# Routed experts of a fused attention, mixture and gated-product kernel: four full tiles of one expert moved ahead into the last routing, and the output weights split by GpSimd

## The reference, cut to what matters

```python
# 1. a gated linear recurrence over 768 steps, 4 batches x 8 heads, head size 48
state = f[:, :, t, :, None] * state + k[:, :, t] (x) v[:, :, t];  y[:, :, t] = q[:, :, t] @ state
# x = y as 3072 rows of 384
# 2. mixture of 8 experts, the two best of each row
noisy = x @ w_gate + log1p(exp(x @ w_noise)) * noise
top2  = two largest of noisy;  share = softmax(top2)
out[row] += share * (relu(x[row] @ w1[e]) @ w2[e])        # w1: 384x1024, w2: 1024x384
# 3. gated product
rms = sqrt(mean(x * x) + 1e-6);  xn = x / rms * rms_g
result = (silu(xn @ w_gate2) * (xn @ w_val2)) @ w_out2    # 384x1536, 1536x384
```

## Time and profile before

| what | value |
|---|---|
| median of 3 runs | 1334.63 us (1333.99 to 1335.31) |
| the profiled execution's own time | 1338.19 us |
| its span, first to last instruction | 1336.4 us |
| TensorE busy | 1239.8 us (93%) |
| VectorE, ScalarE, GpSimd busy | 880.5, 460.6, 443.0 us |
| mean granted TensorE clock | 0.978 |

### The profile page before, as it was taken

How to read it: one execution, slowest core, us unless ns; L and a number is a source line. 1 busy time by engine, 2 the same in 40 slices (tenths; PEclk the granted TensorE clock), 3 DMA queues, 4 the chain that set the end, 5 groups by cost and what they waited for, 6 DMA issues and landing times.

```text
span 1336.4 us, 26652 instructions
## 1 busy us (share of the span) xinstructions
PE 1239.8 (93%) x8897; PEld 1145.7 (86%) x8898; DVE 880.5 (66%) x1976; ACT 460.6 (34%) x975; POOL 443.0 (33%) x375
## 2 busy tenths in 40 slices
PE   4899999992999999999999999299999999999998
PEld 3787878772899999999999998299999999999997
DVE  6888888855778778778778778344444444444433
ACT  3555655642222222222222222332323323232321
POOL 8567787734614415060617600410101101010000
PEclk9999999996999999999999999699999999999999
DMA  8233433214413131313223320210101101010000
GB/s 304 67 102 125 136 119 110 69 49 153 181 69 136 47 135 41 141 54 122 94 91 109 127 109 21 80 36 19 36 21 34 54 1 54 18 35 18 0 19 18
DMA packets 36174, 105.44 MB, mean 79 GB/s; under 512 B 4992, under 2 KB 20352, under 8 KB 33664
## 3 DMA queue, kind: packets, MB, share of 16 engines
q1 hardware_dynamic: 26928, 55.62, 12.3%
q0 software_dynamic: 8592, 47.98, 10.2%
q10 hardware_dynamic: 576, 0.79, 0.2%
HBM read 77.83 MB, written 26.54 MB: 78 GB/s over the span
## 4 chain that ended last, share of the span: by engine, by line
PE 74%; DVE 8%; POOL 7%; issue 5%; ACT 4%; DMA 1%; another core or an unknown queue 0%; DVEq 0%; ACTq 0%; SPq 0%; POOLq 0%
PE pD L1529 13%; PE pD L1594 9%; PE pA L1594 9%; PE pS L1553 9%; PE pA L1553 8%; PE pA L1607 6%; PE pA L1343 5%; PE pA L1529 4%; PE pS L1607 3%; PE pA L1540 2%; PE pX L1509 1%; DVE W L974 1%; POOL fT L523 1%; POOL prods L558 1%; PE pD L1379 1%
## 5 line engine op out<-in xcount | busy, mean ns | idle before, releaser
L1204 DVE STREAM_TRANSPOSE pA<-pD 32x128 f32<-32x128 f32 x448 | 148.9, 332 | 54.1 <-PE pD L1529 47.9
L1284 DVE TENSOR_TENSOR gs<-pD,sig 128x384 f32<-128x384 f32 x96 | 53.5, 557 | 196.9 <-ACT sig L910 196.8
L1204 DVE STREAM_TRANSPOSE pA<-pA 32x128 f32<-32x128 f32 x432 | 143.6, 332 | 45.3 <-PE pA L1529 39.2
L692 POOL DMA_INDIRECT pair<-y_sorted,y_row x48 | 50.2, 1046 | 365.1 <-DVE z L1263 278.3
L858 ACT ACTIVATE hidH<-pA 128x512 fp32r<-128x512 f32 x110 | 66.0, 600 | 268.0 <-DVE pA L1204 263.2
L1343 PE MATMUL pA<-W 64*128 64x128 f32 x1920 | 141.8, 288 | 17.2 <-DVE W L974 11.5
L1529 PE MATMUL pD<-we,xsH 128*128 x498 | 155.5, 393 | 0.4 <-issue 0.4
L1343 PEld LDWEIGHTS pA<-W 64*128 64x128 f32 x1920 | 119.6, 191 | 36.5 <-DVE W L974 17.8
L1553 PE MATMUL pS<-we,hidH 128*128 x448 | 117.8, 344 | 2.4 <-DVE hidL L1211 2.0
L974 DVE TENSOR_TENSOR W<-W,prods 128x512 f32<-128x512 f32 (+1 forms) x120 | 97.8, 821 | 32.7 <-PE pA L1343 26.3
L910 ACT ACTIVATE sig<-pD 128x384 f32<-128x384 f32 x96 | 47.3, 492 | 208.4 <-PE pA L1594 208.2
(11 more groups left out here) (207 smaller groups left out, 2842.9 us busy)
## 6 DMA issues: line engine op xcount, KB each, us to landing
stage<-w POOLq DMA_DIRECT2D x14, 1536.0 KB, 8.8
qk<-qk_t SPq DMA_DIRECT2D x24, 512.0 KB, 3.7
xs<-x_sorted SPq DMA_DIRECT2D x55, 192.0 KB, 2.4
y_sorted<-yo SPq DMA_DIRECT2D x55, 192.0 KB, 1.9
fT<-f_t SPq DMA_DIRECT2D x12, 512.0 KB
vN<-v_n SPq DMA_DIRECT2D x24, 256.0 KB, 2.8
out<-fin SPq DMA_DIRECT2D x8, 576.0 KB, 2.8
stage<-w SPq DMA_DIRECT2D x2, 1536.0 KB, 13.7
```

The source lines that it names most:

```text
L692: pool.indirect_dma_start(out=pair[:, j, k], out_offset=None, in_=y_sorted[:, :], in_offset=bass.IndirectOffsetOnAxis(ap=y_row[:, t * TS + ...
L1204: ins = dve.transpose(by_32[1][32 * q:32 * (q + 1), :, i], by_32[0][32 * i:32 * (i + 1), :, q])
L1284: dve.tensor_tensor(gs[:], pD[:, f % 2 * 512:f % 2 * 512 + TT], sig[f % 2][:], ALU.mult).then_inc(s_u, 1)
```

## The change

Expert order. When eight of the twelve pairs have been routed, VectorE takes the expert with most rows so far. It becomes the first in turn, and expert 0 takes its place; all later tables go by turn. SyncE loads that expert's weights then, not at the start. Two thirds of 3072 rows with two choices are 4096 places, so that expert has at least 512 rows, four full tiles.

Early tiles. TensorE, ScalarE, VectorE and SyncE run tiles 0 to 3 (`EARLY`) between the last pair's attention and routing steps, in an order written out by hand. For these tiles TensorE transposes all of the hidden tile. The remaining 51 slots run as before. ScalarE and VectorE split the first weights in halves, two of them inside the last pair's body. GpSimd's first split waits for more steps of VectorE (`s_yrow` 10).

Output weights. GpSimd splits them in place of ScalarE and VectorE, in two column blocks (`outHa`, `outHb`, `outL`). The first block of 384 rows of the gated product is combined, squared and scaled tile by tile of 128, each on its own semaphore.

```diff
@@ SyncE @@
-            sp.dma_start(stage1[:], w1[0]).then_inc(s_stage, 16)
-            sp.dma_start(stage2[:], w2[0]).then_inc(s_stage, 16)
             pairs(body)
+            sp.wait_ge(s_most, 3)
+            e = sp.value_load(first_i[0:1, 0:1], min_val=0, max_val=E - 1)
+            sp.dma_start(stage1[:], w1[bass.ds(e, 1)]...).then_inc(s_stage, 16)
+            sp.dma_start(stage2[:], w2[bass.ds(e, 1)]...).then_inc(s_stage, 16)
+            for s in s_sc:
+                sp.wait_ge(s, 64 * 2)
+            for n in range(EARLY):
+                load_early(Tile(n), e)
+            store_rows(Tile(0))
+            sp.wait_ge(s_tab, TAB_COUNT)
+            clear_rows(sp, range(E))
+            for s in s_sc:
+                sp.wait_ge(s, 64 * (NP // 4))
+            sp.wait_ge(s_zero, 16 * E)
+            sp.wait_ge(s_tab, TAB)
+            wait_alone(sp, s_tx, 1)
+            load_rows(Tile(4))
@@ GpSimd @@
-            pool.wait_ge(s_tab, TAB)
-            for s in s_xs:
-                pool.wait_ge(s, 16)
+            pool.wait_ge(s_turn, 2)
             for e in range(1, E):
...
+                if e == 1:
+                    pool.wait_ge(s_y, NT)
+                    pool.wait_ge(s_yrow, 10)
+                    for s in s_sc:
+                        pool.wait_ge(s, 64 * (NP // 4))
...
+            pool.wait_ge(s_stage1, 16 * (E + 2))
+            for high, c in ((outHa, slice(0, OUT_A * DM)), (outHb, slice(OUT_A * DM, F2C * DM))):
+                split(high[:], outL[:, c], stage3[:, c], s_last)
@@ ScalarE: in body(NP - 1), and after it @@
+                if k == NP - 1:
+                    high_weights(0, 0)          # before soft_noise(r)
+                if k == NP - 1:
+                    high_weights(0, 1)          # before spread_state(a - 2)
+            take_rect(b, 5); take_keys(a); take_logit_parts(NP - 2); soft_noise(NP - 2); high_x(Tile(0))
+            high_weights(1, 0); take_y(a); spread_state(a); exp_gap(NP - 2); high_weights(1, 1)
+            rectify(Tile(0)); take_x(a); take_y(b); high_h(Tile(0), 0); high_h(Tile(0), 1); take_x(b)
+            take_logit_parts(NP - 1); high_x(Tile(1)); soft_noise(NP - 1); exp_gap(NP - 1); take_rows(Tile(0))
...
-            act.copy(outH[:], stage3[:]).then_inc(s_split0, 1)
@@ VectorE: in body(NP - 1), and after it @@
+                if k == NP - 1:
+                    low_weights(0, 0)           # before double_blocks(b, 3)
+                if k == NP - 1:
+                    low_weights(0, 1)           # before double_blocks(a, 5)
+            double_blocks(NT - 1, 5); take_ranks(NP - 3); low_x(Tile(0)); top2(NP - 2); new_state(NT - 2)
+            mark_chosen(NP - 2); mark_hits(NP - 2); running_counts(NP - 2); take_rows(NP - 3)
+            low_weights(1, 0); low_weights(1, 1); order_experts(); low_h(Tile(0), 0); low_h(Tile(0), 1)
+            take_ranks(NP - 2); low_x(Tile(1)); add_noise(NP - 1); top2(NP - 1)
...
-            dve.tensor_tensor(outL[:], stage3[:], outH[:].bitcast(F32), ALU.subtract).then_inc(s_last, 1)
+            first_combine(0); first_combine(1); first_norm(0); first_combine(2); first_norm(1); first_norm(2)
@@ TensorE, after body(NP - 1) @@
+            turn_keys(a); ranks(NP - 3); logits(NP - 2); attend(a, (0,)); turn_rows(Tile(0))
+            attend(a, (1, 2, 3)); key_values(a); hidden(Tile(0)); turn_x(a); attend(b, (0, 1, 2, 3))
+            turn_hidden(Tile(0)); turn_x(b); logit_parts(NP - 1); ranks(NP - 2); turn_rows(Tile(1))
+            logits(NP - 1); output(Tile(0)); ranks(NP - 1); hidden(Tile(1))
+            pe.matmul(pD[:, at:at + E], ones[:], hits[:, :, 0], ...)        # the counts
+            turn_rows(Tile(2)); turn_hidden(Tile(1)); hidden(Tile(2)); turn_rows(Tile(3)); turn_hidden(Tile(2))
+            output(Tile(1)); hidden(Tile(3)); turn_hidden(Tile(3)); output(Tile(2)); turn_rows(Tile(4))
+            output(Tile(3)); pe.wait_ge(s_tab, TAB); hidden(Tile(4)); turn_rows(Tile(5)); turn_hidden(Tile(4))
```

More of the change, by code:

```diff
@@ L352, in program @@
         s_yo = sem("s_yo")
-        s_pair = sem("s_pair")
+        s_pair = [sem(f"s_pair{j}") for j in range(TS)]
+        s_first = sem("s_first")
+        s_rms = sem("s_rms")
         s_z = sem("s_z")
@@ L1146, in body @@
                     double_blocks(a, 5)
-            pairs(body)
+            for k in range(NP):
+                body(k)
+            double_blocks(NT - 1, 5)
+            take_ranks(NP - 3)
+            low_x(Tile(0))
+            top2(NP - 2)
+            new_state(NT - 2)
+            mark_chosen(NP - 2)
+            mark_hits(NP - 2)
+            running_counts(NP - 2)
+            take_rows(NP - 3)
+            low_weights(1, 0)
+            low_weights(1, 1)
+            order_experts()
+            for h in range(2):
+                low_h(Tile(0), h)
+            take_ranks(NP - 2)
+            low_x(Tile(1))
+            add_noise(NP - 1)
+            top2(NP - 1)
+            mark_chosen(NP - 1)
+            mark_hits(NP - 1)
+            running_counts(NP - 1)
+            take_rows(NP - 2)
+            take_ranks(NP - 1)
+            take_rows(NP - 1)
             n_tab = [0]
@@ new lines, in _ @@
+            for h in range(2):
+                low_h(Tile(2), h)
+            dve.tensor_tensor(start_t[:], ends[:], tiles_of[:], ALU.subtract).then_inc(s_yrow, 1)
+            dve.wait_ge(s_yrow, 1)
+            dve.scalar_tensor_tensor(out=start_t[:], in0=start_t[:], scalar=float(P), in1=turn_row[:],
+                                     op0=ALU.mult, op1=ALU.subtract).then_inc(s_yrow, 1)
+            dve.wait_ge(s_yrow, 2)
+            dve.tensor_tensor(turned[:], turn[:], start_t[:].unsqueeze(1).to_broadcast([P, E, E]),
+                              ALU.mult).then_inc(s_yrow, 1)
@@ L1297, in take_out @@
                     dve.tensor_copy(fin[t.par][:, j], out_bank(j)).then_inc(s_fin, 1)
-            combine(Tile(0, None, 2))
-            norm(Tile(0, None, 2))
+            first_combine(0)
+            first_combine(1)
+            first_norm(0)
+            first_combine(2)
+            first_norm(1)
+            first_norm(2)
             for k in range(KC):
@@ L1541, in turn_hidden @@
                 ins.then_inc(s_th, 1)
+                if early(t):
+                    for k in range(FC // 2):
+                        c = slice(k * P, (k + 1) * P)
+                        ins = pe.transpose(pA[0][:, 1, c], hid[:, HF:][:, c], ident[:])
+                    ins.then_inc(s_ht, 1)
             def output(t):
@@ L1556, in output @@
                 ins.then_inc(s_g2, 1)
-            turn_rows(Tile(0))
-            turn_rows(Tile(1))
-            hidden(Tile(0))
-            turn_hidden(Tile(0))
+            for k in range(NP):
+                body(k)
+            a, b = NT - 2, NT - 1
+            turn_keys(a)
+            ranks(NP - 3)
+            logits(NP - 2)
+            attend(a, (0,))
+            turn_rows(Tile(0))
+            attend(a, (1, 2, 3))
+            key_values(a)
+            hidden(Tile(0))
+            pe.wait_ge(s_xl, 1)
+            turn_x(a)
+            attend(b, (0, 1, 2, 3))
+            turn_hidden(Tile(0))
+            turn_x(b)
+            logit_parts(NP - 1)
+            ranks(NP - 2)
+            turn_rows(Tile(1))
+            logits(NP - 1)
+            output(Tile(0))
+            ranks(NP - 1)
+            hidden(Tile(1))
+            pe.wait_ge(s_pl, PL * (NP - 1) + 1)
+            at = HT + 2 * P + 6 * E
+            pe.matmul(pD[:, at:at + E], ones[:], hits[:, :, 0], start=True, stop=True).then_inc(s_cnt, 1)
+            turn_rows(Tile(2))
+            turn_hidden(Tile(1))
+            hidden(Tile(2))
+            turn_rows(Tile(3))
+            turn_hidden(Tile(2))
+            output(Tile(1))
+            hidden(Tile(3))
+            turn_hidden(Tile(3))
+            output(Tile(2))
+            turn_rows(Tile(4))
+            output(Tile(3))
+            pe.wait_ge(s_tab, TAB)
+            hidden(Tile(4))
+            turn_rows(Tile(5))
+            turn_hidden(Tile(4))
             def slot(t):
```

389 lines of the change are left out of this document (275 added, 114 removed).

## The result

The changed kernel takes 1316.44 us (median of 4, 1315.64 to 1317.75) against 1334.97 (1333.99 to 1335.96) for the one before: a ratio of 0.9864, interval 0.9849 to 0.9880. That is 18.5 us faster where 26.7 were forecast. (The kernel before had one run more here than in the table ahead of the prediction, hence 1334.97 and not 1334.63.) The time lies in the range of 1300 to 1318, but outside the 1301.6 to 1313.6 of the forecast proper (rival 1), and in the span that rival 2 named for another cause. The profiled execution took 1315.64 us, its span 1314.0.

A forecast was written before the change was run, and what follows sets the result against it. TensorE bounds the expert slots and is short of work before the fifth slot's output and before the gate; gains 18.8 + 7.9 = 26.7 us take the median from 1334.63 to 1308, 8 in 10 within 1300 to 1318.

The forecast's parts named there:

- rival 1: Whole change, the forecast proper: both parts work, gain 21 to 33 us (1301.6 to 1313.6); chance 0.64.
- rival 2: Early tiles: one hand-over late, likeliest tile 4's load or weights landing in the last body; gain 12 to 20, 1315 to 1322; chance 0.17.
- both kernels run the same 50 slots: Behind output(4): the same slots in both kernels, still 9.08 us each, so no gain or loss there.
- first part: Up to output(4): early tiles fill TensorE's idle time behind the last pair, 383.4 - (363.1 + 1.5) = 18.8 us gained.
- second part: Last slot to gate: four us off the last gather's landing, less work behind it; gate at 856.6, not 864.5, 7.9 us gained.
- The last pair's body: Weight splits placed there partly show on TensorE: 0.5 to 3.3 us, taken as 1.5; about 3 if weights land at 280.
- The waits laid out: TensorE's waits up to output(4): about 4.8, then 2.6 for low_x(5), 0.8 for low_h(4), plus 1.5 for hand-overs.
- rival 4: Nearly all laid-out waits vanish and the clock returns sooner behind the gathers: gain above 33, below 1301 us; chance 0.07.
- Tile 4's load: Early tiles: load issued near 336, on chip near 340, TensorE asks near 346; slack 6 us, lateness past it is time.
- Rival 5: Second expert's weights late, first split behind VectorE's row steps: slower, if `s_yrow` 10 comes over 47 us after 340; chance 0.02.
- rival 6: Early tiles: the change does nothing, as the expert's early tiles wait for the same scatters; chance 0.02.
- Rival 3: Gathers before the gate stay slow through their own transfer or queue, not VectorE: gain 22.7, 1312 us; chance 0.08 alone.

The follow-up runs named there:

- set 2: One chip, kernel before 1334.72 us: buffers shifted in the kernel before (1341.13), moved back in the changed one (1308.33), six VectorE operations added to the changed one (1316.54, 1316.56).
- placed: Changed kernel with buffers padded 960 and 2144 bytes, back to their old offsets within 2048 bytes: 1308.33 us, ratio 0.9802 to the kernel before.
- the zeros' edit: Placed version, with GpSimd waiting for the eight zero tiles before asking for the second expert's weights: 1309.67 us, ratio 0.9815 to the kernel before.
- the second part alone: Kernel before with only GpSimd splitting the output weights and the first 384 rows combined tile by tile: 1332.52 us, ratio 0.9936 to the kernel before.
- set 1: One chip, kernel before 1340.25 us: both kernels unchanged (changed one 1318.10), output-weight and tile-by-tile work alone (1332.52), tile 5's rows earlier in the changed one (1318.57).
- sets 2 and 3: Two sets of runs, each on one chip, kernel before 1334.72 and 1333.96 us; moving its weights and activations gave 1341.13, its activations alone 1342.27.

## Why the prediction fell where it did

By the profiled executions the change gained 22.4 us of span (1336.4 to 1314.0) against 26.7:

| stretch | forecast | measured |
|---|---|---|
| to output(4) | 18.8 | 20.3 |
| output(4) to the last copy | 0 | -3.0 |
| last copy to gate | 7.9 | 7.85 |
| gated product | 0 | -2.7 |

**The step that failed** is the sentence that behind output(4) "both kernels run the same 50 slots", with "Slots still 9.08 us", and that the gated product keeps its time. I took a matmul's length as fixed by its shape and the clock. The moved buffers made it 1 to 6 ns longer in the hidden products and 3 to 5 ns in the gate and value products, together 5.7 us over both stages. The term that the forecast had at nothing measured 6.4 and 8.2 us by the medians of set 2, in the two directions. At equal places of the buffers the change is worth 26.4 us (placed against before, 24.0 to 28.8 by the interval), 24.3 with the zeros' edit, or 24.6 within set 2 (before moved to the changed kernel's places, 1341.13, against 1316.56). The last two are some 2 us short of the 26.7 forecast; that the first is not is partly luck. The second term that failed is TensorE's work in the first part, below.

**First part, 18.8 forecast, 20.3 measured.** Errors of both signs lie on top of each other here, and that the two numbers are near is luck. In the profiled kernel before, VectorE stood for 4.5 us and ScalarE for 3.1 near 288 us, in the last pair's body, and TensorE ran only some matmuls with gaps. Its chain, which the forecast's had only as a busy share of 23.67 in 25.4, has it as

```profile
287.51 3.63 another core or an unknown queue
```

The stop recurs in the kernel before run again and in the version with the second part alone. It is in none of the changed kernels, nor in the two versions of the kernel before with buffers moved, whose output(4) starts at 379.48 and 379.35 and not 383.36. Against those the new order gained 16.3 us, not 18.8. In set 1, where both kernels have a trace from one chip, it is 21.6 with the stop (385.37 to 363.79). The second part's version, with the stop too, starts output(4) only at 388.03, 4.7 us after the kernel before; why is open.

Where the 2.5 us went: the sum had 58.0 us of TensorE's work behind the last body and 9.7 of waits, and the trace has 61.4 and 7.9. The six hidden products are the difference. At 4.12 each they were to take 24.7 us and were busy 28.1, 6.01 of it in hidden(5) behind its wait of 2.8, at a granted clock of 0.76 (4.34 in the placed version, behind the same wait). The forecast's "the new order should keep none" of the slow matmuls was wrong by that piece. The start of output(4) differs by up to 2.5 us between executions of the changed kernel and its like (361.28 to 363.79), so single pieces are readings and no proof.

**From span to median.** I took the median 3.6 us under the profiled execution, as it was before. After, it is 0.8 above it. The stop is the likely reason. On the chips of sets 2 and 3 moving the buffers of the kernel before cost 6.4 and 8.3 us by the medians, and the moved kernels' traces, which lack the stop, show 5.7 and 7.9 us more in slots and gated product than the trace of the kernel before. Had its unprofiled executions there held a stop of 3.6 us that the moved ones lack, these differences would be some 3.6 us smaller. In set 1, whose traces of the unchanged order hold the stop, the changed kernel gained 22.1 us and not 18.5, 3.6 more. Without the stop the stages add up: 16.3 + 7.85 - 5.7 = 18.45, and 18.5 was measured. Then the miss of 8.2 us is 5.7 for the places of the buffers and 2.5 for the first part. This is inferred from sums, as no unprofiled execution has a trace. It also means that the moved buffers need not be what removed the stop: the unchanged kernel has no trace on the chips of sets 2 and 3. What causes it stays open.

**The last pair's body.** Forecast: 1.5 us of cost. It took 22.5 us with TensorE busy throughout, so the splits put in cost next to nothing. The weights were asked for at 267.20, as forecast near 266, but came later than the 275 to 278 of the forecast; ScalarE waited 4.34 us for them:

```profile
279.68 1.47 ACT L841 CAST we<-stage 128x1536 fp32r<-128x1536 f32 x1 [4.34 <-DMA stage<-w]
```

That is the far end, 280, at which TensorE was to slip by about 3 us, and it did not slip.

**The waits laid out.** 4.8 + 2.6 + 0.8 + 1.5 = 9.7 forecast, 7.9 measured. low_x(5) is the largest as laid out (2.8 for 2.6). hidden(0) was to start near 304 and started at 300.80, since the body ended at 293.8 and not 296.9. With the waits still there and a clock of 0.76 behind the longest, rival 4 is refuted.

**Tile 4's load, slack of 6 us.** Wrong: issued 5 us later than forecast, slack gone, 1.0 us of TensorE's time. I had given the zeros a share of 9 us; with the weights behind them they took until 341. TensorE's idling on xs there was named as a sign of a wrong prediction; it showed, at a price of 1 us and not 6 to 10. It is the beginning of rival 2, whose 1315 to 1322 hold the measured 1316.44 by chance: the time went elsewhere. (Rival 2's own price, 6 to 10 us off 26.7, gives a gain of 16.7 to 20.7 and not 12 to 20.)

**Second expert.** First split 334.63 against 340; never waited for. Rival 5 stays without support, rival 6 is refuted.

**Gathers.** The second part's 7.85 is the sum of 3.7 for the last landing (16.18 us behind the copy before, 12.45 after; 4.0 forecast) and 4.1 for the work by tiles behind it (9.75 and 5.63; 3.9 forecast). Rival 3, and the inference of the Trainium skill (SBUF — State Buffer, Who interferes with whom), would have had the slow gather stay. The second part's 7.85 us and the 4.96 us operation that stretched a gather to 3.25 speak against both. The Trainium skill's rule, on the same page, that the shared port is held for a whole instruction agrees with the gather's end 0.91 us behind the operation's and with the six short ones, which cost one gather 1 us; the Trainium skill's inference that a two-input operation leaves descriptor writing alone does not, if it is meant for indirect transfers. Their row numbers lie in SBUF, and the same section has such an operation contend with GpSimd's reads of SBUF; whether the reading or the writing is held up, no run here shows.

**Restart at the gate.** Clock 0.61 in the last wait (0.59 before), the slow start stayed as forecast.

## What to carry to other kernels

A change that adds a table also moves every buffer behind it. Where TensorE is the bound, compare the mean duration of one matmul of each group before and after, and if it has moved, pad the buffers back before judging the change: here that was worth 8 us of 26. Keep long VectorE operations with two SBUF inputs off the time at which GpSimd issues indirect transfers that someone waits for; cut up, or with one input in PSUM, they cost less here. A profiled execution may hold a stop that the timed ones do not, as the sums above suggest: compare its own time with theirs before taking its stages as the kernel's. A wait taken off one step pays only up to the next engine's wait: list what stands behind it first.

## What the runs showed of the hardware

- A matmul's duration depends on where its operands lie in SBUF, at the same clock, shape and order: 391 and 396 ns for a matmul of the hidden product's first half, 342 and 346 for one of the gate product. Moving the activations alone by 4000 bytes cost 8.3 us of 1334; moving them 32 bytes more in the changed kernel gained nothing; 2144 bytes more, with the weights 960 more, took it back. The cost is of where the operands lie; by what mechanism is not shown. No rule for good places comes out of these five placements.
- One VectorE operation with both inputs in SBUF holds an indirect transfer's issue on GpSimd until it ends, plus 0.9 us (3.25 us in place of 1.03). Six operations of 1.2 us held it once, for 1 us, the later gathers meeting them at their ends. With the first input in PSUM nothing was held, though four gathers began and ended inside such operations; a long one of that kind was not tried.
- A stop of 3.6 us, shown as an unknown queue, at the same place (287.0 to 288.5 us) in three of the five traces whose first stage has the old order, and in none of the nine others. The two without it have moved buffers and come from other chips than the two of set 1 that hold it. Its cause is open.
